# The down products of a fused attention and mixture kernel, taken half a row of the model's width at a time

## What is computed

```python
p_packed = sm_attn(p, k, v)
out = sm_attn(q, p_packed, p_packed)       # 4608 tokens x 512
# dense layer
h = x @ w_in                               # 512 -> 1024
solu = h * softmax(h)
ln = (solu - mean(solu)) / sqrt(var(solu) + 1e-06) * g_ln
y = ln @ w_out                             # 1024 -> 512: the down product
# experts
expert_idx = argmax(y @ w_gate, axis=1)
out[token] = gate_w * (relu(y @ w1[e]) @ w2[e])
```

## Time and profile before

| | before |
|---|---|
| median of 3 runs | 1053.02 us (1052.04 to 1053.51) |
| the profiled execution, its own time | 1053.62 us |
| its span in the trace | 1051.9 us |
| PE busy | 994.8 us, 95% |
| PEld busy | 797.3 us, 76% |
| DVE, ACT, POOL busy | 513.2, 439.6, 287.3 us |
| mean granted clock of PE, share of full speed | 0.967 |

### The profile page before, as it was taken

How to read it: one execution, slowest core, us unless ns; L and a number is a source line. 1 busy time by engine, 2 the same in 40 slices (tenths; PEclk the granted TensorE clock), 3 DMA queues, 4 the chain that set the end, 5 groups by cost and what they waited for, 6 DMA issues and landing times.

```text
span 1051.9 us, 19962 instructions
## 1 busy us (share of the span) xinstructions
PE 994.8 (95%) x5708; PEld 797.3 (76%) x5709; DVE 513.2 (49%) x1228; ACT 439.6 (42%) x767; POOL 287.3 (27%) x638
## 2 busy tenths in 40 slices
PE   7658999999999999999989799999999999999994
PEld 4337777777787777877878688888888888888883
DVE  3446666766666666767754632234252523422221
ACT  2344556565565555655562422133142513311220
POOL 1430222322222222245563222122221212221120
PEclk9658999999999999999999899999999999999997
DMA  9212222122232221431114731124161421111110
GB/s 355 81 57 70 91 82 91 31 91 91 91 100 81 68 65 41 146 106 42 40 32 121 280 120 40 50 79 160 42 207 40 158 92 40 40 45 44 40 43 27
DMA packets 64760, 92.63 MB, mean 88 GB/s; under 512 B 42944, under 2 KB 45120, under 8 KB 64704
## 3 DMA queue, kind: packets, MB, share of 16 engines
q1 hardware_dynamic: 55584, 61.96, 18.5%
q0 software_dynamic: 9120, 29.97, 8.4%
HBM read 70.37 MB, written 21.54 MB: 87 GB/s over the span
## 4 chain that ended last, share of the span: by engine, by line
PE 90%; DVE 2%; ACT 2%; issue 2%; POOL 1%; DMA 1%; POOLq 0%; SPq 0%; ACTq 0%; DVEq 0%
PE ps L1417 39%; PE ps L1503 13%; PE ps L1424 8%; PE ps L1482 7%; PE ps L1510 6%; PE ps L1491 3%; PE ps L1453 3%; PE ps L1382 2%; PE ps L1531 2%; PE ps L1339 2%; PE ps L1359 2%; PE ps L1348 1%; POOL w_in L454 1%; PE ps L1301 1%; DMA qb<-y_sorted 1%
## 5 line engine op out<-in xcount | busy, mean ns | idle before, releaser
L1417 PE MATMUL ps<-W,zr 128*128 (+1 forms) x912 | 221.2, 399 | 2.6 <-DVE zr L1145 2.6
L1417 PE MATMUL ps<-W,xr 128*128 (+1 forms) x912 | 219.4, 396 | 2.8 <-POOL small L580 2.8
L1417 PEld LDWEIGHTS ps<-W,zr 128*128 128x128 f32 x912 | 171.4, 191 | 37.4 <-issue 2.8
L1417 PEld LDWEIGHTS ps<-W,xr 128*128 128x128 f32 x912 | 169.5, 189 | 37.3 <-DVE xr L1140 2.8
L1503 PE MATMUL ps<-w_out,zr 128*128 128x512 f32 x576 | 146.8, 405 | 0.0
L1503 PEld LDWEIGHTS ps<-w_out,zr 128*128 128x128 f32 x576 | 102.6, 188 | 29.3 <-issue 6.9
L831 ACT ACTIVATE zr<-ps 128x1024 fp32r<-128x1024 f32 x38 | 39.0, 1026 | 193.5 <-PE ps L1424 193.5
L471 POOL TENSOR_TENSOR small<-half 128x1 f32<-128x1 f32 x78 | 24.1, 309 | 323.7 <-DVE yb L1157 187.0
L1157 DVE TENSOR_SCALAR yb<-ps,gate 128x512 f32<-128x512 f32 x38 | 28.5, 751 | 131.8 <-PE ps L1417 131.7
L1140 DVE TENSOR_TENSOR xr<-ps,xr 128x512 fp32r<-128x512 f32 x39 | 26.9, 691 | 132.8 <-ACT xr L821 131.7
L826 ACT ACTIVATE hbuf<-ps 128x1024 f32<-128x1024 f32 x38 | 38.8, 1021 | 126.2 <-PE ps L1417 126.2
(11 more groups left out here) (224 smaller groups left out, 1493.7 us busy)
## 6 DMA issues: line engine op xcount, KB each, us to landing
raw_e<-w_exp SPq DMA_DIRECT2D x48, 512.0 KB, 5.5
qb<-y_sorted POOLq DMA_DIRECT2D x40, 257.0 KB, 3.0
vb<-v_t SPq DMA_DIRECT2D x16, 640.0 KB, 5.5
kb<-k_t SPq DMA_DIRECT2D x16, 576.0 KB, 4.5
qb<-q_t SPq DMA_DIRECT2D x144, 64.0 KB, 3.3
y_sorted<-pad SPq DMA_DIRECT2D x8, 257.0 KB, 3.7
raw_out<-w_moe SPq DMA_DIRECT2D x4, 512.0 KB, 5.1
raw_in<-w_moe SPq DMA_DIRECT2D x4, 512.0 KB, 14.3
```

Source lines behind the costliest of these rows:

```text
L1417: mm = nc.tensor.matmul(dst, lhs[:, a, k * P:(k + 1) * P], rhs(b, cols), start=(first and n == 0), stop=(last and n == 2))
```

## The change

`down_hi` and `down_lo` get a half. A matmul now streams 256 columns of `w_out` in place of 512, so each chunk of `zr` is loaded once for each half, and there are 48 matmuls and 48 loads a tile in place of 24 and 24. The first half of the columns is finished, remainder products and all, before the second is begun.

```diff
-            def down_hi(t, chunks):
-                if chunks[0] == 0:
+            def down_hi(t, half, chunks):
+
+                cols = slice(half * D // 2, (half + 1) * D // 2)
+                if chunks[0] == 0 and half == 0:
                     pe.wait_ge(z_hi_done, t + 1)
...
                 for k in chunks:
                     for part in range(2):
-                        nc.tensor.matmul(y_ps, zr[:, 0, k * P:(k + 1) * P], w_out[:, part, k * D:(k + 1) * D],
+                        nc.tensor.matmul(y_ps[:, cols], zr[:, 0, k * P:(k + 1) * P],
+                                         w_out[:, part, k * D:(k + 1) * D][:, cols],
                                          start=(k == 0 and part == 0), stop=False)
 
-            def down_lo(t, chunks):
-                if chunks[0] == 0:
+            def down_lo(t, half):
+                cols = slice(half * D // 2, (half + 1) * D // 2)
+                if half == 0:
                     pe.wait_ge(z_lo_done, t + 1)
-                for k in chunks:
-                    mm = nc.tensor.matmul(y_ps, zr[:, 1, k * P:(k + 1) * P], w_out[:, 0, k * D:(k + 1) * D],
-                                          start=False, stop=(k == KF - 1))
-                if chunks[-1] == KF - 1:
+                for k in range(KF):
+                    mm = nc.tensor.matmul(y_ps[:, cols], zr[:, 1, k * P:(k + 1) * P],
+                                          w_out[:, 0, k * D:(k + 1) * D][:, cols], start=False, stop=(k == KF - 1))
+                if half == 1:
                     mm.then_inc(y_product, 1)
...
                     logits_t(t - 1)
-                    down_hi(t - 1, range(0, 4))
+                    down_hi(t - 1, 0, range(0, KF))
                     turn_logits(t - 1)
-                    down_hi(t - 1, range(4, KF))
+                    down_lo(t - 1, 0)
+                    down_hi(t - 1, 1, range(0, 2))
                 if v is not None:
                     m_half(v, 1)
...
                 if there(t - 1):
-                    down_lo(t - 1, range(0, 4))
+                    down_hi(t - 1, 1, range(2, KF))
...
                 if there(t - 1):
-                    down_lo(t - 1, range(4, KF))
+                    down_lo(t - 1, 1)
```

More of the change, by code:

```diff
@@ L1644, in _ @@
             e_turn_x(1)
-            down_hi(NT - 1, range(KF))
+            down_hi(NT - 1, 0, range(KF))
+            down_lo(NT - 1, 0)
             rank(NT - 1)
-            down_lo(NT - 1, range(KF))
+            down_hi(NT - 1, 1, range(KF))
+            down_lo(NT - 1, 1)
             pe.wait_ge(pick_chain, 4 * (NT - 1) + 1)
```

## The result

The changed kernel takes 1057.75 us (median of 5 runs, 1057.31 to 1060.73) against 1053.02; the ratio is 1.0055, with a 95% interval of 1.0039 to 1.007. A second series of it, further down, gave 1.0049 (1.0036 to 1.0063). So it is half a per cent slower. The profiled execution took 1059.52 us, 5.9 more than that of before.

What follows compares the result with a forecast made beforehand. PE was taken to bound the kernel: two halves at 118 ns make 236 against 231, 5 ns more x 864 = +4.3 us. 1053.6 + 4.3 = 1057.9, with the median 0.6 lower: 1057.3 us, range 1047 to 1070.

Steps and rivals of the forecast that it cites:

- PE is the bound, each nanosecond counts: Steady stretch: PE busy 465.49 of 471.00 us, so a nanosecond of PE in the down product is one of the kernel.
- The floor of the load, 112 ns from the rows of L1453: Down product: a 128x128 load and changeover take 112 ns, just fitting under a half matmul of 116 to 118.
- The stream in proportion, 0.4375 ns a column: Half matmuls of the down product: 256 columns stream in 112 ns, and the next starts after 116.
- the second rival: Slower: a price for each fp32r matmul, 125 ns a half in the down product, +16.4 us, 1069.4; chance 0.25.
- The 3 ns of the down bursts, halved for each half: Down bursts run at 231 ns, not 228; half of these 3 ns added per half matmul: 117.5, rounded to 118.
- Moved places at nothing: The `z_lo_done` wait, L1382, `k_turn`, `turn_a`, `y_product` and the last tile's ranks change place or timing; all costed at nothing.
- the wait for `z_lo_done`: Now ahead of the first half's remainder products; PE asks 1.5 us after it is there, so no cost.
- The first rival: Faster: loads alone set the down product's pace, 112 ns a half, 224 against 231, -6.0 us, 1047.0; chance 0.13.
- the third: Rival: cover fails, each load stands beside its half matmul in the down product, 224 ns a half, +187 us, 1240; chance 0.04.
- The fourth rival: Nothing to be measured: down product at 115 to 117 ns a half, 230 to 233 against 231; chance 0.2.
- What the profile was to show: Down product: 16 halves in 1.9 us, 8 in 0.94, durations near 277 ns; no PE wait at L1514 or L1348.

Runs made afterwards that it cites:

- The ladder: Changed kernel with a row's two parts at unequal widths, 128+384 to 256+256 columns, by tile number modulo 6; 1070.27 us, ratio 1.0165.
- the order alone: Kernel before, with whole rows of 512 columns in the places the change gave the halves, nothing split; 1051.9 us, ratio 0.9998.

## Why the prediction held

The time was 1057.75 for 1057.3 predicted. The sign and the place were right; that the size came out so close is in part luck, since the price behind it was wrong, in two terms that partly made up for each other. Step by step:

- **PE is the bound, each nanosecond counts.** Held: +6.3 us of starts in the down product became +6.3 from its first matmul to its last. The medians rose by 4.7 and 5.1 us; both intervals (4.1 to 7.4 and 3.8 to 6.6 us) hold 6.3.
- **The floor of the load, 112 ns from the rows of L1453.** Held within 1 ns, at five widths. The load still fits beside 256 columns, with 8 ns to spare where the prediction had 5. The Trainium skill ("TensorE: Matmul & The Clock Gate", on what overlaps and what doesn't) states that a weight load overlaps matmuls in flight only when its group of rows is another one. The ladder speaks against it for this kernel: 240 columns, 100 ns at 0.417 a column, and a load of all 128 rows, 105 to 108, come together every 112 ns.
- **The stream in proportion, 0.4375 ns a column.** This was the step that failed. It took the 165 ns of a duration that don't depend on the width from plain f32; for fp32r they are 177, by the durations of 512 and 256 columns. The settled starts show 0.417 ns a column and 13.3 ns for each matmul, which is the mechanism of the second rival. The prediction's 116 for the steady pace was 4 too low.
- **The 3 ns of the down bursts, halved for each half.** Halves came at 118.7 to 120.0 from the second place on, nowhere slower than when settled; so this term, 1.5 and rounded to 2, stood for nothing that was there, and happened to make up for half of the one before. 118 was taken, 119.5 measured: 239 a pair in place of 236, 8 x 864 = +6.9 us by these paces and +6.3 by the sum of starts, in place of +4.3. So the sum was 2.0 us too small, and the median, which rose by less than the starts did, fell closer to it.
- **The second rival, +16.4 us.** Its mechanism was right and its price too high: it charged all of 231 - 213 = 18 ns to the matmul. Of these 13.3 are the price, seen in the settled part; the other 4.6 are what whole rows take more, on average, in the first dozen places behind a break, and halves didn't pay them.
- **Moved places at nothing.** Held within about 1 us, by the order alone at 0.9998. For the wait for `z_lo_done`, in the pass of the earlier trace rows, DVE ends at 486.86 + 1.23 = 488.09 and the load of the first remainder product starts at 489.47, 1.4 us later (1.5 foreseen; the smallest of the 36 tiles is 1.34):

```profile
486.86 1.23 DVE L1059 TENSOR_TENSOR zr<-zraw,zr 128x1024 fp32r<-128x1024 f32 x1 [0.22 <-ACT zraw L757]
489.47 1.01 PEld L1514 LDWEIGHTS ps<-w_out,zr 128*128 128x128 f32 x8
```

- **The first rival (the load's pace, faster) and the third (no cover).** Neither came. The load sets the pace at 240 columns and below, 16 fewer than a half has; but two such parts don't make a row of 512.
- **The fourth rival (nothing to be measured, 115 to 117 ns a half).** It lay 2.5 ns under the 119.5 measured, and both intervals of the ratio exclude 1.
- **What the profile was to show.** The duration was 283 ns and not 277, the groups 1.92 and 0.95 for 1.9 and 0.94; no wait of PE for DVE or ACT at the new places, as foreseen. (The one wait of L1348 for ACT in the stretch, 2.15 us at 88.33, stands ahead of the first down product and was 2.15 us before.)

## What to carry to other kernels

In this kernel a matmul in the settled part of a burst costs the larger of two sums: its load, 112 ns for 128x128 in four bytes, or a fixed price and its columns, 13.3 ns and 0.417 each. Splitting in two costs one fixed price for each matmul added as long as each part stays above the load's floor, and below it each part costs the full floor. In short bursts the split costs less than that, here 6.3 us in place of 11.5, because wide matmuls lose some ns in each of the first dozen places behind a break and narrower ones don't.

Two widths in a trace are needed to tell a price for each column from a price for each matmul. With one width, carry both as cases, don't borrow the fixed part of a duration from another type, and look for the floor in the narrow matmuls of the same kernel. And compare paces at the same place behind a break: the average over short bursts hid here what the settled part shows.

## What the runs showed of the hardware

- The change from one bound to the other is sharp: 240 columns every 112 ns, 256 every 120. The fixed price alone would make 113 of 240 columns.
- Whole rows of fp32r take 228 to 238 ns from start to start in the places 2 to 10 behind a break, on average by place, and 226.7 from the sixteenth on, in the products of the kernel before. Halves take 118 to 120 throughout.
- Plain f32 pays less for each matmul than fp32r. The chain of before has, at a granted clock of 1.00, 16 matmuls of 512 columns in f32 (8 calls of the program, each of which stands in the trace twice):

```profile
12.61 6.87 PE ps L1301 x16
```

  429 ns each, with a duration of 592; with the 0.833 ns a column taken from the durations, 427 of columns and 2 more. A settled fp32r matmul takes 13.3 more than its columns, at half the time for a column. No run here tells why.
- Narrower loads change the pace of 256-column matmuls by a few ns and not in order of size: 119 to 120 at 128 columns of weights, 116 at 64, 118 at 32.
